# A two-layer perceptron behind a dynamic convolution: VectorE takes over all low halves of g in the second tile, the third tile is transposed by DMA, and the first tile's preparation is reordered

## The reference

```
# x (4, 4096, 192), weight_gen (4, 4096, 8, 7), w_in (192, 2048), w_out (2048, 192), all float32
w = softmax(weight_gen, axis=-1)
x_pad = 6 rows of zeros, then x, along the sequence
a[b, s, h*24+g] = sum over k < 7 of w[b, s, h, k] * x_pad[b, s+k, h*24+g]
h = a.reshape(16384, 192) @ w_in
g = maximum(0.01*h, h)
out = g @ w_out
```

## Time and profile before

| What | Before |
|---|---|
| median of 3 runs | 1070.72 us (1069.48 to 1070.96) |
| the profiled execution, its own time | 1068.83 us |
| its span (first to last instruction) | 1066.9 us |
| TensorE busy | 1052.1 us, 99% |
| TensorE's weight loads | 721.1 us |
| VectorE busy | 778.0 us, 73% |
| ScalarE busy | 634.4 us, 59% |
| GpSimd busy | 485.3 us, 45% |
| granted TensorE clock, mean | 0.999 |

### The profile page before, as it was taken

One profiled execution on the slowest core, in us unless ns is written; L12 is line 12 of the kernel. 1 busy time (PEld: TensorE's weight loads), 2 busy tenths in 40 slices (PEclk: granted clock), 3 DMA queues, 4 the chain that ended last, 5 costly groups with the idle time before them and its releaser, 6 DMA issues.

```text
span 1066.9 us, 20802 instructions
## 1 busy us (share of the span) xinstructions
PE 1052.1 (99%) x8799; PEld 721.1 (68%) x8799; DVE 778.0 (73%) x1098; ACT 634.4 (59%) x1335; POOL 485.3 (45%) x381
## 2 busy tenths in 40 slices
PE   8999999999999999999999999999999999999998
PEld 3566666766766766776676676676676677667666
DVE  7998968687577877758677577876768777586711
ACT  6766556655555655565665565655566565566554
POOL 0055544544454554454454354454445444445433
PEclk9999999999999999999999999999999999999999
DMA  9100212104031021212202131030311212111010
GB/s 257 55 23 16 78 34 74 51 17 94 18 93 33 25 85 33 79 33 40 83 20 85 27 94 33 15 94 18 93 33 31 79 33 78 33 33 32 17 33 16
DMA packets 65845, 56.57 MB, mean 53 GB/s; under 512 B 54684, under 2 KB 58908, under 8 KB 63768
## 3 DMA queue, kind: packets, MB, share of 16 engines
q1 hardware_dynamic: 65628, 54.95, 18.6%
q10 hardware_dynamic: 124, 0.29, 0.1%
HBM read 29.34 MB, written 12.58 MB: 39 GB/s over the span
## 4 chain that ended last, share of the span: by engine, by line
PE 91%; DVE 7%; ACT 1%; issue 0%; DMA 0%; DVEq 0%; ACTq 0%
PE out_ps L837 30%; PE out_ps L843 15%; PE h_ps L797 10%; PE h_ps L798 10%; PE h_ps L796 10%; PE h_ps L795 10%; PE h_ps L811 6%; DVE conv L534 2%; DVE prod L527 2%; DVE gl L576 1%; PE h_ps L893 1%; ACT xs L364 0%; ACT g L379 0%; ACT gh L377 0%; DMA taps<-in_weight_gen_dram 0%
## 5 line engine op out<-in xcount | busy, mean ns | idle before, releaser
L252 POOL TENSOR_TENSOR gl<-g,gh 128x512 f16<-128x512 f32 x372 | 483.2, 1327 | 573.8 <-ACT g L379 573.8
L377 ACT ACTIVATE gh<-h_ps 128x512 f16<-128x512 f32 x512 | 317.5, 620 | 383.7 <-PE h_ps L814 383.7
L837 PEld LDWEIGHTS out_ps<-wo,gh 128*128 128x128 f16 x4064 | 329.0, 98 | 54.4 <-issue 53.4
L837 PE MATMUL out_ps<-wo,gh 128*128 128x192 f16 x4064 | 359.4, 246 | 0.5 <-DVE wo L556 0.5
L576 DVE TENSOR_TENSOR gl<-g,gh 128x512 f16<-128x512 f32 x140 | 128.7, 926 | 265.0 <-ACT g L379 265.0
L379 ACT ACTIVATE g<-h_ps 128x512 f32<-128x512 f32 x512 | 321.8, 628 | 0.0
L534 DVE TENSOR_TENSOR conv<-conv,prod 128x768 f32<-128x768 f32 x186 | 233.0, 1253 | 1.1
L527 DVE TENSOR_TENSOR prod<-xbuf,taps 128x768 f32<-128x768 f32 x186 | 207.0, 1125 | 0.0
L843 PE MATMUL out_ps<-wo,gl 128*128 128x192 f16 x2032 | 189.9, 246 | 2.6 <-DVE gl L576 2.4
L795 PE MATMUL h_ps<-xT,whA 128*128 128x512 f16 x500 | 189.5, 379 | 2.7 <-DVE wlD L556 1.9
L798 PE MATMUL h_ps<-xT,whA 128*128 128x512 f16 x500 | 189.5, 379 | 0.0
(11 more groups left out here) (82 smaller groups left out, 423.6 us busy)
## 6 DMA issues: line engine op xcount, KB each, us to landing
xbuf<-in_x_dram SPq DMA_DIRECT2D x15, 1344.0 KB, 6.0
out_dram<-stage SPq DMA_DIRECT2D x31, 384.0 KB, 2.3
taps<-in_weight_gen_dram SPq DMA_DIRECT2D x16, 224.0 KB, 6.0
xT_again<-xT SPq DMA_DIRECT2D x29, 64.0 KB, 2.1
rawO<-in_moe_w_out_dram SPq DMA_DIRECT2D x4, 384.0 KB, 10.1
rawA<-in_moe_w_in_dram SPq DMA_DIRECT2D x2, 512.0 KB, 8.6
xbuf<-in_x_dram SPq DMA_DIRECT2D x2, 384.0 KB, 7.1
rawD<-in_moe_w_in_dram SPq DMA_DIRECT2D x1, 512.0 KB, 7.0
```

The lines of the kernel that those rows point to most:

```text
L252: nc.gpsimd.tensor_tensor(gl[:, f % RING, :], g[:, f % RING, :], gh[:, f % RING, :], ALU.subtract).then_inc(s_gl_p, 1)
L377: nc.scalar.activation(gh[:, f % RING, :], h_ps[f % GROUP][:], ACT.Prelu, scale=SHRINK, alpha=SLOPE).then_inc(s_gh, 1)
L837: nc.tensor.matmul(out_of(m, j), gh[:, f % RING, j * P:(j + 1) * P], wo[:, f, part, :], start=f == 0 and (j % 2 == 0 or alone) and part == ...
```

## The change

There are four edits. (1) `BY_PE` is 2 instead of 3: the third tile (tile 2) is transposed by SP's DMA, not by TensorE. (2) `EARLY` = 2: in the second tile (tile 1) VectorE makes all 16 lo of g, and GpSimd begins with the third. VectorE's program for the second tile is written out (`second_tile`) instead of coming from `step`. (3) hi of x of the second tile is transposed between the hi and the lo half of project(2), not after it, and ScalarE copies it out in the middle of leaky(3). (4) In the first tile, ScalarE's `split_hi` of pieces ("A", 1) and ("D", 1) stands ahead of `abs_wo(2)` and `abs_wo(3)`, and VectorE's `split_lo` of them ahead of `convolve(1, 1)` and `w_top(1)`.

The two constants, which of VectorE and GpSimd makes a lo of g, and GpSimd's program:

```diff
-        BY_PE = 3
+        BY_PE = 2
+        EARLY = 2
...
         def lo_on_vector(q):
-            return q < NF or q % GROUP == GROUP - 1
+            return q < EARLY * NF or q % GROUP == GROUP - 1
...
-            for q in range(NF, TILES * NF):
+            for q in range(EARLY * NF, TILES * NF):
                 if not lo_on_vector(q):
                     lo_of_g(q, q % NF)
```

ScalarE, its steps and then the first tile:

```diff
-                if i == NG - 1 and m + 1 < BY_PE:
-                    for b in range(2):
-                        take_transposed(m + 1, b)
+                if n == 3:
+                    take_transposed(1, 1)
...
-                if n + 1 < NG * TILES:
+                if n == 2:
+                    leaky(3, 0, 2)
+                    take_transposed(1, 0)
+                    leaky(3, 2, GROUP)
+                elif n + 1 < NG * TILES:
                     leaky(n + 1)
...
             take_transposed(0, 1)
+            for piece in PIECES[2:4]:
+                split_hi(piece)
             for n in range(2, N_PIECES):
                 abs_wo(n)
-            for piece in PIECES[2:4]:
-                split_hi(piece)
```

VectorE, the first tile, the second tile (`-` lines are the end of `first_tile`), and the call:

```diff
-                conv1(0, 2)
+                conv1(0, 1)
+                lo_pieces(2, 4)
+                conv1(1, 2)
                 w_top(1)
                 conv1(2, 3)
-                lo_pieces(2, 4)
                 w_scales(1)
...
+            def second_tile():
                 for n in range(4):
                     convolve(2, n)
-                lo_of_g(NF + GROUP - 1, GROUP - 1)
-                for n in range(4, CONV_AHEAD):
+                group(NG)
+                for n in range(4, 9):
                     convolve(2, n)
+                group(NG + 1)
+                for n in range(9, N_CONV):
+                    convolve(2, n)
+                group(NG + 2)
+                lo_of_x(2)
+                for n in range(6):
+                    convolve(3, n)
+                group(NG + 3)
+                for n in range(6, CONV_AHEAD):
+                    convolve(3, n)
...
-            for n in range(NG, NG * TILES):
+            second_tile()
+            for n in range(2 * NG, NG * TILES):
                 step(n)
```

TensorE, in `project(n)` between the two halves, and in `step(n)`:

```diff
+                if n == 2:
+                    transpose_hi(1)
...
-                if i == NG - 1 and m + 1 < BY_PE:
-                    hidden_by_pe(m + 1)
+                if n + 1 == NG:
+                    hidden_by_pe(1)
                 elif n + 1 < NG * TILES:
                     hidden(n + 1)
...
-                if i == NG - 2 and m + 1 < BY_PE:
-                    transpose_hi(m + 1)
```

More of the change, by code:

```diff
@@ L591, in step @@
                     for k in range(CONV_IN[i]):
-                        if n == NG and k == 2:
-                            lo_of_g((n + 1) * GROUP + GROUP - 1, (n + 1) % NG * GROUP + GROUP - 1)
+                        if n == 2 * NG and k == 2:
+                            lo_of_g(n * GROUP + GROUP - 1, GROUP - 1)
                         convolve(m + 1, CONV_AHEAD + sum(CONV_IN[b] for b in range(i)) + k)
@@ L600, in step @@
                     for k in range(CONV_AHEAD_IN[i]):
-                        if k == (1 if m > 1 else 0):
+                        if k == 1:
                             lo_of_g(n * GROUP + GROUP - 1, n % NG * GROUP + GROUP - 1)
                         convolve(m + 2, sum(CONV_AHEAD_IN[b] for b in range(2, i)) + k)
-                        if n == 2 * NG - 2 and k == 1:
-                            take_transposed(2)
-                elif n > NG + 1:
+                elif n > 2 * NG:
                     lo_of_g(n * GROUP + GROUP - 1, n % NG * GROUP + GROUP - 1)
@@ L658, in conv1, with group @@
                     convolve(1, n)
-            def group0(i):
-                for f in range(i * GROUP, (i + 1) * GROUP):
-                    lo_of_g(f, f)
+            def group(n):
+                for f in range(n % NG * GROUP, (n % NG + 1) * GROUP):
+                    lo_of_g(n // NG * NF + f, f)
             def first_tile():
@@ L682, in first_tile @@
                 conv1(4, 5)
-                group0(0)
+                group(0)
                 lo_pieces(5, 7)
@@ L687, in first_tile @@
                 conv1(9, 11)
-                group0(1)
+                group(1)
                 lo_pieces(8, 10)
@@ L692, in first_tile @@
                 lo_of_x(1)
-                group0(2)
+                group(2)
                 lo_pieces(11, 12)
@@ L698, in first_tile @@
                 take_transposed(1)
-                group0(3)
+                group(3)
                 for n in range(2, N_SOFTMAX):
@@ L818, in wait_lo @@
             def wait_lo(m, f):
[L819 to L822, removed]
+                if m < EARLY:
+                    pe.wait_ge(s_gl_v, m * NF + f + 1)
+                elif lo_on_vector(m * NF + f):
+                    pe.wait_ge(s_gl_v, EARLY * NF + ((m - EARLY) * NF + f) // GROUP + 1)
                 else:
-                    pe.wait_ge(s_gl_p, ((m - 1) * NF + f) // GROUP * (GROUP - 1) + f % GROUP + 1)
+                    pe.wait_ge(s_gl_p, ((m - EARLY) * NF + f) // GROUP * (GROUP - 1) + f % GROUP + 1)
             def project(n):
```

## The result

| | before | changed |
|---|---|---|
| median | 1070.35 us (6 runs, 1069.18 to 1070.96) | 1063.32 us (6 runs, 1062.76 to 1064.30) |
| profiled execution | 1068.83 us | 1063.15 us |
| its span | 1066.9 us | 1061.3 us |

What follows compares the result with a forecast made beforehand. TensorE bounds the kernel, with gains only ahead of 120 us; -0.90 - 2.39 + 0.40 - 2.62 + 0.75 = -4.76 us, from the three-run median 1070.72 us to 1065.9 us. Range 1063.6 to 1068.8 us.

Steps and rivals of the forecast that it cites:

- the three waits: TensorE's excess ahead of 120 us: after project(2), in the 10.45 us step from 83.60, in the 10.68 us step from 102.11.
- edit 3, hi of x inside project(2): Between project(2) and hidden_by_pe(1): transposes fit into an existing wait and ScalarE's copy wait goes, -0.90 us (-1.07 to -0.5).
- edit 1, transposes gone: Third tile on TensorE: twelve transposes and the wait for their copies go, step 10.45 to 8.06 us, -2.39 us.
- edit 1, xT late at hidden(8): At hidden(8): DMA-transposed xT lands at 87.07 us, TensorE arrives at 86.67, +0.4 us (nothing to 1.4).
- edit 2, the wait of 2.45 us gone: At project(8): VectorE, without GpSimd beside it, is in time with its gl; step 10.68 to 8.06 us, -2.62 us.
- edit 4, ScalarE waits for rawD: First tile: ScalarE asks for piece ("D", 1) before its data land, waits 0.80 us and delays what follows, +0.75 us.
- The charge of 0.17 us: In hidden_by_pe(1): its fourth product waits for ScalarE's later last g, 0.17 us, between nothing and 0.57 us.
- A: First tile's ("D", 1) data are there and xT is just in time: -5.5 to -5.9 us, 1065.0 us, chance 0.17.
- B: At hidden(8), xT and xT_again both come late, 1.0 + 0.8 us more: -3.0 us, 1067.7 us, chance 0.13.
- C: VectorE stays late in the third tile beside GpSimd, the 2.62 us stay: -2.1 us, 1068.6 us, chance 0.08.
- D: DMA latency shows in full, hidden(8) waits 4.3 us in place of 0.4: -0.9 us, 1069.8 us, chance 0.06.
- E: VectorE bounds the second tile, slow at 1.80 us without GpSimd, TensorE waits for xT: about +7 us, 1078 us, chance 0.03.

Runs made afterwards that it cites:

- second profile: The changed kernel run and profiled once more with no edit: median 1063.43 us over five runs, ratio 0.9936 to before.
- the twins with GpSimd in the second tile: Changed kernel with GpSimd again making three of four second-tile lo of g: 1067.41 us; the same with hidden(8)'s wait filled by 12 unread products: 1066.12 us.

## Why the prediction was right and where it was wrong

The direction was right and the three waits went; the gain was 2.3 us larger than forecast (7.03 us, not 4.76). The time was 2.6 us shorter, since the median of before's six runs is also 0.4 us below the 1070.72 us of three. The terms, on TensorE's timeline:

| step of the prediction | predicted | first profile | second profile | the step alone undone |
|---|---|---|---|---|
| edit 3, hi of x inside project(2) | -0.90 | -1.05 | -1.06 | 1.05 |
| edit 1, transposes gone | -2.39 | -2.39 | -2.39 | 1.44, the rest is edit 2's |
| edit 1, xT late at hidden(8) | +0.40 | +0.08 | +0.08 | |
| edit 2, the wait of 2.45 us gone | -2.62 | -2.62 | -2.62 | the wait moves to hidden(8): 2.73 us |
| edit 4, ScalarE waits for rawD | +0.75 | +0.35 | -0.11 | project(2) as late as in before, 29.83 us |
| sum | -4.76 | -5.63 | -6.10 | |

Edit 1's two terms are the step 82.90 to 91.04, 8.14 us, against 8.06 without a wait and 10.45 before.

- *Edit 3.* The charge of 0.17 us for ScalarE's later g did not come: hidden_by_pe(1) to project(3) is 4.55 us after and 4.54 before.
- *xT at hidden(8).* Lo of x ended when SP issued its transpose, at 83.14, close to the 82.77 forecast. The landing was taken at 4.3 us, from the first one in the earlier trace rows; it took 3.77, close to the median of the earlier trace rows.
- *Edit 2* went as argued: the second tile's products are at 0.95 us, and the experiment with GpSimd busy shows why.
- *Edit 4* was sized from one landing, 9.3 us in the one profile of before, and put at +0.75. The wait for rawD was 0.36 us in one profile and none in six others, where the edit gains 0.1 us.

In the first profile the mis-sized terms are 0.40 + 0.32 + 0.15 = 0.87 us, nearly all of the 0.92 us by which the changed kernel's profiled execution (1063.15) lies under the 1064.07 of the sum. The rest, 1.7 us, is the step that failed: "that execution was 1.89 us under the median of the three runs, and against the median, 1070.72 us, it is 1065.9 us" (1066.0 by its own numbers). It carried the distance over as if it would stay, into the forecast and into the range, whose lower end is a rival's time counted from the same median. It was no offset but **a second price of the wait that edit 2 removes**: in 20 of 34 runs of before the time is at the upper level, and the two profiles taken there have the lower clock behind this wait, for 1.6 to 1.7 us. The profile that was read had none of it. In the terms of the sum, edit 2 is worth 2.62 us in a short execution of before, and 12.37 - 8.06 = 4.31 and 12.28 - 8.06 = 4.22 us in the two long ones; the sum had the lower clock at nothing. With the wait gone, the price goes too, which is why the changed kernel's profiled time and median are 0.2 us apart. Counted from the median of before's lower level, 1069.2 us, the sum of the second profile gives 1063.1 us; 1063.32 and 1063.43 were measured. The filled wait in before shows it best; the twins with GpSimd in the second tile show the same price, but two of the filled runs were long all the same. Why the clock falls behind the same wait in one execution and not in another stays open.

Of the rivals, A's conditions are nearly what most profiles show: rawD was there in six of seven, and xT came 0.08 us late in both profiles of the changed kernel. Its -5.5 to -5.9 us is close to the -6.1 of the second profile; its time, 1065.0 us, is 1.7 us too long by the same offset. B, C, D and E did not come.

## What to carry to other kernels

Before a profile's distance from the median is carried over as an offset, look at the spread of the runs: two levels can be a cost that the profile does not contain. A mean granted clock under 1 says that the clock fell, but neither where nor whether it cost anything: 0.998 stands beside runs of both levels here, and only the stretches of a long execution's profile show the place. A wait of some 2.5 us on TensorE can cost the wait and, behind it, a stretch at the lower clock; filling it with products that nobody reads can tell the two apart. Terms read from one timeline can overlap: undoing each edit by itself gave 1.4 us for one that the sum had at 2.4, because another edit paid for the rest.

## What the runs showed of the hardware that was not expected

- Behind one and the same wait of 2.45 us TensorE's granted clock fell to about 0.5 in two profiles of before and stayed at 1.00 in five; it cost 1.60 and 1.69 us.
- In the first profile of the changed kernel the clock was 0.50 from 28.0 to 31.4 us (the first stretch above), behind idle times of 1.43 and 0.47 us, and one long profile of before has 0.52 there. It does not show in the end, since project(2) waits for VectorE anyway: in that profile of before it came 29.83 us after the first transposes, as in those without the fall.
- GpSimd working on data of its own slowed the VectorE instructions that ran beside it: a 128x768 product from 0.96 to 1.80 us, and a set of four lo of g from 2.49 to 4.41 us.
